# GpSimd instead of VectorE forms two low parts ahead of the first value product

## The chip, the cores and the metric

The kernel runs on one core of one Trainium2 chip. The metric is device time in microseconds; "before" took 577.25 us as the median of three runs (576.12 to 578.04). All data is float32.

## The reference

Three stages follow each other on 4 batches of 768 tokens with 384 features (8 heads of 48). The part that matters here is the start of the second stage, whose input x is the result of the first.

```python
for t in range(S):                                   # stage 1: decayed linear attention
    state = alpha[:, :, t, :, None] * state + np.einsum('bhd,bhe->bhde', k[:, :, t], v[:, :, t])
    y[:, :, t] = np.einsum('bhd,bhde->bhe', q[:, :, t], state)
x = y.transpose(0, 2, 1, 3).reshape(B, S, H * D)

for k in range(K):                                   # stage 2: gate by 5 taps along time, and a value
    gate_pre += conv_w[k][None, None, :] * xp[:, k:k + S, :]
gate = 1.0 / (1.0 + np.exp(-gate_pre))
val = x @ w_val                                      # the product whose operands the change touches
x2 = gate * val @ w_out

u = x2 + np.real(fft(fft(x2, axis=1), axis=2))       # stage 3: Fourier mixing, norm, MLP
un = (u - mean) / np.sqrt(var + 1e-06)
out = u + np.maximum(un @ w_ch1, 0.0) @ w_ch2
```

## The kernel before, in words

Products that need more precision than one pass gives are split. For an operand `a`, ScalarE writes a high part `a_hi` (a copy into the type fp32r), VectorE writes the low part `a_lo = a - a_hi`, and TensorE adds three products: high by high, high by low, low by high. `w_hi`, `w_lo` and `w_raw` hold the weights (`w_lo` lies in the place of `w_raw`), `x_hi` and `x_lo` the input x in two halves of 384 tokens, each 128 partitions by 3 x 384 = 1152 elements.

One list, `SCHEDULE`, sets the order. Every engine walks it and issues its own share of each step; the engines meet only at semaphores, which count. The list is written by hand: `prologue()` for the attention of the first batch, then for each batch `front(b)` (value product, gate, Fourier mixing) and `mlp(b)`, into which the next batch's attention is woven. The attention runs in 6 chunks of 128 tokens. For each chunk VectorE scans the decays forward (`load`, L803) and backward (`inv`, L814), scales k and q (`scale`, L820 and L821, giving `kd` and `qd`), masks the scores that TensorE has made (`mask`, L827) and updates the state (`state`, L835 and L838). TensorE makes the `scores` from `kd` and `qd` (L960), turns the keys (L969), sums the chunk (L980) and forms `y` from the old state (L998) and the masked scores (L1003). ScalarE copies `y` to `xT` (L637).

In `prologue()`, chunk 3 has ScalarE's `whi` of the value weights (L587) and `xhi` of x's first half (L640). VectorE's counterparts come later in its order: `("wlo", 0, 0, 0)` in chunk 4, behind the scales of chunk 5 and the state of chunk 4 (L867), and `("xlo", 0, 0, 0)` in chunk 5, behind that chunk's masks (L870). Between and behind them VectorE adds taps of the gate (`tapv`, L856 and L859). The high and low parts of x's second half follow at chunk 5's end. The first readers are the steps `("val", 0, 0, 0)` and `("val", 0, 1, 0)` of `front(0)` (L1060), which wait for `s_xhi`, `s_xlo` and, for the weights, `s_wlo` through `weight_ready`. `WLO_AT` gives a weight step's number in the count of `s_wlo`.

GpSimd has little to do before: it builds the identity and the mask (L524 to L530), waits until five chunks of x are there, issues the loads of the cosine and sine tables (L536), and then issues all stores (L543). SyncE issues the other loads. TensorE also forms gate taps as products (`tapj`, L1046) and `wd`, the product of the output weights with a Fourier matrix (L1052).

Of the kernel before, what the change touches and what calls it, by code (L numbers as in the profile page):

```python
# [5 lines left out]
F32 = mybir.dt.float32  # L6
F32R = mybir.dt.float32r
ALU = mybir.AluOpType
# [9 lines left out]
HALF = S // 2  # L18
# [4 lines left out]
PAD = TAPS - 1  # L23
# [180 lines left out]
def order_of(*kinds):  # L204

    return {w: j for j, w in enumerate(w for w in SCHEDULE if w[0] in kinds and not (w[0] == "pair" and w[2] > 0))}
# [8 lines left out]
            for w, j in order_of("val", "u", "vlo", "oddrow", "pair", "comb", "t", "h", "out").items()}  # L215
for b_ in range(B):
    DREAD_AT["pqe", b_, 0, 0] = DREAD_AT["pqo", b_, 0, 0]
WHI_AT, WLO_AT = order_of("whi"), order_of("wlo")

def bank_plan():
# [35 lines left out]
def build(nc, q, k, v, alpha, w_val, conv_wt, w_out, w_out_t, w1, w2, dft_d, fold_cos, fold_nsin, odd_col, odd_row, out):  # L257
    ctx = ExitStack()
    with ctx:
        def sb(name, shape, dt=F32):  # L260
            return ctx.enter_context(nc.sbuf_tensor(name, shape, dt))

        def sem(name):
            return ctx.enter_context(nc.semaphore(name))
# [9 lines left out]
        def at(name, shape, dt, offset):  # L274
            return nc.alloc_sbuf_tensor_at(name, shape, dt, offset=offset)
# [3 lines left out]
        w_hi, w_lo, w_raw = {}, {}, {}  # L279
# [12 lines left out]
        x_hi = [at(f"x_hi{h}", [128, K, HALF], F32R, z1 + (2 - 2 * h) * HALFB) for h in range(2)]  # L292
        x_lo = [at(f"x_lo{h}", [128, K, HALF], F32R, z1 + (3 - 2 * h) * HALFB) for h in range(2)]
# [13 lines left out]
        def slot(t):  # L307

            m, mirrored = divmod(t, 2)
            return 2 * m + 2 if mirrored else max(2 * m - 1, 0)  # L310
# [34 lines left out]
        xT = sb("xT", [128, K, PAD + S])  # L345
# [39 lines left out]
        def part(t, i, j):  # L385

            if WN[i] == "w1":
                return t[:, :, j * FF // 3:(j + 1) * FF // 3]
            if WN[i] == "w2":
                return t[:, j, :]  # L390
            return t[:, :, :].rearrange("p k n -> p (k n)")
# [25 lines left out]
        s_diag = sem("diagonals_ready")  # L417
        s_whi = sem("weights_hi")
        s_wlo = sem("weights_lo")

        s_in = [sem("qk_loaded_even"), sem("qk_loaded_odd")]
        s_ain = [sem("alpha_loaded_even"), sem("alpha_loaded_odd")]
# [17 lines left out]

        s_xhi = sem("x_hi_ready")
        s_xlo = sem("x_lo_ready")
        s_tap = sem("taps_added")
        s_tap0 = sem("first_tap_ready")
        s_tapv = sem("first_batch_taps_added")
# [26 lines left out]
        def read(w):  # L472
            return DREAD_AT[w] + 1
# [48 lines left out]
        @block.gpsimd  # L522
        def _(pool):
            pool.memset(ident[:, :], 0.0).then_inc(s_zero, 1)  # L524
            pool.wait_ge(s_zero, 1)
            pool.affine_select(out=ident[:, :], in_=ident[:, :], compare_op=ALU.not_equal, fill=1.0, base=0,
                               pattern=[[-1, 128]], channel_multiplier=1).then_inc(s_consts, 1)
            pool.wait_ge(s_sets, 6)

            pool.affine_select(out=mask[:, :], in_=mask[:, :], compare_op=ALU.is_ge, fill=0.0, base=0,  # L530
                               pattern=[[1, 128]], channel_multiplier=-1).then_inc(s_consts, 1)

            pool.wait_ge(s_xc, NCH - 1)
            for name, table in (("cos", fold_cos), ("nsin", fold_nsin)):
                for dst, part_ in ((w_hi[name], 0), (w_lo[name], 1)):
                    pool.dma_start(dst[:, :, :], table[part_]).then_inc(s_wload[WN.index(name)], 16)  # L536

            for w in SCHEDULE:
                kind, b, a, f = w
                if kind == "out":  # L540
                    t = a * TG + f
                    pool.wait_ge(s_read, read(w))
                    pool.dma_start(out[b, t], u[:, slot(t), :]).then_inc(s_out, 16)  # L543
            pool.wait_ge(s_out, 16 * STORES * B)
# [3 lines left out]
        def _(act):  # L548
# [19 lines left out]
            for w in SCHEDULE:  # L568
                kind, b, a, f = w
# [61 lines left out]
                elif kind == "y":  # L631
                    act.wait_ge(s_y, b * NCH + a + 1)
                    if a == 0 and b > 0:
                        wait_for(act, s_tap, (b - 1) * 2 * (TAPS - 1) * K)
                        act.wait_ge(s_xlo, 2 * b)
                    here = slice(PAD + a * CH, PAD + (a + 1) * CH)
                    act.activation(xT[:, :, here], ys[:, :, :], ACT.Copy).then_inc(s_xc, 1)  # L637
                elif kind == "xhi":
# [48 lines left out]
        def _(dve):  # L687
# [102 lines left out]
            for w in SCHEDULE:  # L790
                kind, b, a, f = w
# [58 lines left out]
                elif kind == "tapv":  # L850
# [6 lines left out]
                    else:  # L857
                        dve.wait_ge(s_tapv, a * TAPS + f)
                        dve.scalar_tensor_tensor(acc, xT[:, m, first + f:end + f], wconv[:, m, f:f + 1], acc,  # L859
                                                 ALU.mult, ALU.add).then_inc(s_tapv, 1)  # L860
                elif kind == "wlo":
                    dve.wait_ge(s_whi, WHI_AT["whi", 0, a, f] + 1)
                    raw, high, low = (part(w_[WN[a]], a, f) for w_ in (w_raw, w_hi, w_lo))
                    if WN[a] == "wout":
                        dve.scalar_tensor_tensor(low, raw, 0.5, high.bitcast(F32), ALU.mult, ALU.subtract).then_inc(s_wlo, 1)
                    else:
                        dve.tensor_tensor(low, raw, high.bitcast(F32), ALU.subtract).then_inc(s_wlo, 1)  # L867
                elif kind == "xlo":
                    dve.wait_ge(s_xhi, 2 * b + a + 1)
                    dve.tensor_tensor(x_lo[a][:, :, :], xT[:, :, PAD + a * HALF:PAD + (a + 1) * HALF],  # L870
                                      x_hi[a][:, :, :].bitcast(F32), ALU.subtract).then_inc(s_xlo, 1)
# [53 lines left out]
        def _(pe):  # L925
# [20 lines left out]
            def weight_ready(name, j=0):  # L946

                pe.wait_ge(s_wlo, WLO_AT["wlo", 0, WN.index(name), j] + 1)
# [77 lines left out]
            for w in SCHEDULE:  # L1026
                kind, b, a, f = w
# [32 lines left out]
                elif kind == "val":  # L1060
                    if a == 0:
                        pe.wait_ge(s_xhi, 2 * b + f + 1)
                        pe.wait_ge(s_xlo, 2 * b + f + 1)
                    if w == ("val", 0, 0, 0):
                        weight_ready("wval")
                    product(ps[:, 0:HALF], [(w_hi["wval"][:, k_, cols], w_lo["wval"][:, k_, cols],
                                             x_hi[f][:, k_, :], x_lo[f][:, k_, :]) for k_ in range(K)]).then_inc(s_unit, 1)
                elif kind == "u":
# [168 lines left out]
```

## Time and profile before

| | before |
|---|---|
| median of 3 runs | 577.25 us (576.12 to 578.04) |
| the profiled execution, its time | 579.33 us |
| its span, first to last instruction | 577.5 us |
| TensorE (PE) busy | 556.3 us |
| VectorE (DVE) busy | 387.9 us |
| ScalarE (ACT) busy | 211.8 us |
| GpSimd (POOL) busy | 16.2 us |
| mean granted TensorE clock | 0.99 |

All times inside the kernel are microseconds from the start of the span. A row of a timeline gives the start, the duration, the engine, the line of the kernel, the operation, output and inputs, the shape, the count of merged instructions, and in brackets the idle time of the engine before it with what ended it. "PEld" is TensorE's weight load, "issue" time without a wait that the profile shows. TensorE's instruction ends are modelled, so its rows overlap; starts are the safer numbers. The granted clock is a share of 2.4 GHz: 1.00 is 2.4 GHz and 0.50 is 1.2 GHz.

### The profile page before, as it was taken

To read this page: it belongs to the slowest core of one execution; us is meant where nothing else is said; L and a number is where in the kernel's file an instruction comes from. 1 tells how busy PE (TensorE), PEld (TensorE's weight loads), DVE (VectorE), ACT (ScalarE), POOL (GpSimd) and SP (SyncE) were. 2 spreads that over 40 slices of the span, in tenths; PEclk is the share of its full clock that TensorE was granted. 3 is DMA by queue.
4 is the path that set the end of the run, shared out by engine and by line. 5 is a ranking of instruction groups with operands and counts; after the bars stand their busy time and mean duration, and the time that the engine had idled before them with its cause. 6 is when DMAs were issued, how large, how long until landed. Compare 5 with 4: busy or idle time off the path is not lost.

```text
span 577.5 us, 13430 instructions
## 1 busy us (share of the span) xinstructions
PE 556.3 (96%) x5623; PEld 530.0 (92%) x5623; DVE 387.9 (67%) x858; ACT 211.8 (37%) x482; POOL 16.2 (3%) x35
## 2 busy tenths in 40 slices
PE   5999999999999999999999999999999999999995
PEld 4887998899999998998999999999999999999995
DVE  7798888978848686877847476886935474552221
ACT  5354364534352135335252134335334134322210
POOL 0001000000000000000000000000000000000000
PEclk9699999999999999999999999999999999999999
DMA  7668301232302000222202001132000000000000
GB/s 254 190 217 294 99 14 44 72 93 63 92 30 57 29 15 28 75 59 86 59 28 59 28 1 42 32 89 87 15 1 28 28 0 2 1 1 28 27 1 27
DMA packets 16234, 34.60 MB, mean 60 GB/s; under 512 B 3312, under 2 KB 6640, under 8 KB 15920
## 3 DMA queue, kind: packets, MB, share of 16 engines
q1 hardware_dynamic: 13632, 27.20, 15.8%
q0 software_dynamic: 2112, 6.29, 3.1%
q8 instruction: 44, 0.72, 0.5%
q10 hardware_dynamic: 432, 0.27, 0.1%
q14 instruction: 14, 0.11, 0.1%
HBM read 29.03 MB, written 4.72 MB: 58 GB/s over the span
## 4 chain that ended last, share of the span: by engine, by line
PE 84%; DVE 7%; ACT 4%; issue 2%; DMA 1%; DVEq 0%; POOL 0%; ACTq 0%
PE bank L933 41%; PE bank L1018 23%; PE evens L960 3%; PE bank L1003 3%; PE bank L998 2%; PE bank L1046 2%; PE sums L969 2%; PE bank L1117 2%; PE sums L980 1%; PE bank L1083 1%; PE bank L1127 1%; PE bank L1052 1%; DVE w_lo L867 1%; DMA oddr_raw<-in_odd_row_dram 1%; DVE unT_lo L690 1%
## 5 line engine op out<-in xcount | busy, mean ns | idle before, releaser
L915 DVE SCALAR_TENSOR_TENSOR h_lo<-bank,h_hi 128x256 fp32r<-128x256 f32 x144 | 60.5, 422 | 106.6 <-ACT h_hi L683 102.1
L933 PE MATMUL bank<-unT_hi,w_hi 128*128 128x256 f32 x432 | 125.1, 290 | 4.5 <-DVE unT_lo L690 2.4
L933 PE MATMUL bank<-unT_lo,w_hi 128*128 128x256 f32 x432 | 122.0, 283 | 0.0
L933 PE MATMUL bank<-unT_hi,w_lo 128*128 128x256 f32 x432 | 121.6, 281 | 0.0
L683 ACT ACTIVATE h_hi<-bank 128x256 fp32r<-128x256 f32 x144 | 54.7, 381 | 164.0 <-PE bank L933 164.0
L1018 PE MATMUL bank<-w_hi,h_hi 128*128 128x384 f32 x288 | 99.9, 347 | 0.0
L1018 PE MATMUL bank<-w_lo,h_hi 128*128 128x384 f32 x288 | 97.6, 339 | 0.0
L1018 PE MATMUL bank<-w_hi,h_lo 128*128 128x384 f32 x288 | 97.3, 338 | 0.0
L933 PEld LDWEIGHTS bank<-unT_hi,w_hi 128*128 128x128 f32 x432 | 81.2, 188 | 9.6 <-DVE unT_lo L690 5.0
L933 PEld LDWEIGHTS bank<-unT_hi,w_lo 128*128 128x128 f32 x432 | 81.6, 189 | 0.0
L933 PEld LDWEIGHTS bank<-unT_lo,w_hi 128*128 128x128 f32 x432 | 81.5, 189 | 0.0
L1018 PEld LDWEIGHTS bank<-w_hi,h_hi 128*128 128x128 f32 x288 | 54.1, 188 | 2.2 <-issue 0.4
L1018 PEld LDWEIGHTS bank<-w_lo,h_hi 128*128 128x128 f32 x288 | 54.1, 188 | 0.0
L1018 PEld LDWEIGHTS bank<-w_hi,h_lo 128*128 128x128 f32 x288 | 54.1, 188 | 0.0
L848 DVE SCALAR_TENSOR_TENSOR gate<-xT,wconv,gate 128x384 f32<-128x384 f32 x72 | 42.3, 611 | 0.4
L960 PEld LDWEIGHTS evens<-qd,kd 48*128 48x128 f32 x192 | 24.0, 193 | 6.8 <-issue 5.1
L814 DVE TENSOR_TENSOR_SCAN kd<-a_in,ends 128x516 f32<-128x516 f32 x24 | 29.6, 1233 | 0.8
L960 PE MATMUL evens<-qd,kd 48*128 48x128 f32 x192 | 28.6, 291 | 1.5 <-DVE qd L821 1.4
L803 DVE TENSOR_TENSOR_SCAN lam<-a_in,starts 128x516 f32<-128x516 f32 x24 | 29.4, 1224 | 0.9 <-DMA a_in<-in_alpha_dram 0.8
L960 PE MATMUL odds<-qd,kd 48*128 48x128 f32 x192 | 28.6, 291 | 0.0
L543 POOL DMA_DIRECT2D out_dram<-u x24 | 12.9, 541 | 513.2 <-DVE u L921 513.2
L1003 PE MATMUL bank<-scores,v_in 128*32 128x128 f32 (+1 forms) x768 | 26.7, 282 | 0.0
(185 smaller groups left out, 1043.4 us busy)
## 6 DMA issues: line engine op xcount, KB each, us to landing
v_in<-in_v_dram SPq DMA_DIRECT2D x24, 224.0 KB, 2.7
w_raw<-in_w_dram SPq DMA_DIRECT2D x2, 2304.0 KB, 10.5
out_dram<-u POOLq DMA_DIRECT2D x24, 192.0 KB, 2.3
a_in<-in_alpha_dram SPq DMA_DIRECT2D x44, 96.9 KB, 2.2
q_in<-in_q_dram SPq DMA_DIRECT2D x44, 96.0 KB, 2.2
k_in<-in_k_dram SPq DMA_DIRECT2D x44, 96.0 KB, 2.3
dftd<-in_dft_d_dram SPq DMA_DIRECT2D x1, 582.0 KB, 4.4
wval_raw<-in_w_val_dram SPq DMA_DIRECT2D x1, 576.0 KB, 5.5
```

The costliest lines, as they stand in the source:

```text
L543: pool.dma_start(out[b, t], u[:, slot(t), :]).then_inc(s_out, 16)
L683: act.activation(h_hi[:, f % HBUF, :], ps[:, 0:GW], ACT.Relu).then_inc(s_hi, 1)
L803: dve.tensor_tensor_scan(lam_[:, :, :].rearrange("d p t -> d (p t)"), a_t[:, 0:NP * CW], starts[:, :, :].rearrange("d p t -> d (p t)"), 0. ...
L814: dve.tensor_tensor_scan(kd_[:, :, :].rearrange("d p t -> d (p t)")[:, ::-1], a_t[:, NP * CW:0:-1], ends[:, NP * CW:0:-1], 0.0, ALU.mult, ...
L848: dve.scalar_tensor_tensor(acc, xT[:, m, t + a * HALF:t + (a + 1) * HALF], wconv[:, m, t:t + 1], acc, ALU.mult, ALU.add).then_inc(s_tap, 1)
L915: dve.scalar_tensor_tensor(h_lo[:, f % HBUF, :], ps[:, 0:GW], 0.0, h_hi[:, f % HBUF, :].bitcast(F32), ALU.max, ALU.subtract).then_inc(s_re ...
L933: last = pe.matmul(ps, l, r, start=(i == 0), stop=(i == len(mms) - 1))
L960: last = pe.matmul(ps[:, p, :], kd_[rows, p, 1:CW], qd_[rows, p, :], start=True, stop=True)
L969: last = pe.transpose(sums[:, p, :], tokens(kd_)[:, p, :], ident[:, :])
L998: pe.matmul(ys[32 * p:32 * p + 32, x, :], st[:, p, first:first + width], qd_[:, p, :], start=(x == 0), stop=False, skip_group_check=True)
L1003: last = pe.matmul(ys[32 * p:32 * p + width, x, :], v_[:, p, first:first + width], scores[:, e, p, :], start=(c == 0 and x == 0), stop=Tru ...
L1018: last = pe.matmul(ps, l[:, f % HBUF, rows], r, start=(f == 0 and x == 0), stop=(f == NF - 1 and x == 2))
```

## The change

The two steps `("wlo", 0, 0, 0)` and `("xlo", 0, 0, 0)` leave VectorE. GpSimd issues the same two subtractions of 128 x 1152 elements right after its mask and ahead of its wait for the table loads: the first when `s_whi` reaches 1, the second when `s_xhi` reaches 1. Each has a semaphore of its own (`s_vallo`, `s_xlo0`), since the counts of `s_wlo` and `s_xlo` are now without them; `WLO_AT` leaves the one step out, and the waits for `s_xlo` count one less. The first val product waits for the two new semaphores in place of the old ones. All other low parts stay with VectorE.

```diff
--- before.py
+++ after.py
@@ -215,7 +215,8 @@
             for w, j in order_of("val", "u", "vlo", "oddrow", "pair", "comb", "t", "h", "out").items()}
 for b_ in range(B):
     DREAD_AT["pqe", b_, 0, 0] = DREAD_AT["pqo", b_, 0, 0]
-WHI_AT, WLO_AT = order_of("whi"), order_of("wlo")
+WHI_AT = order_of("whi")
+WLO_AT = {w: j for j, w in enumerate(w for w in order_of("wlo") if w != ("wlo", 0, 0, 0))}
 
 
 def bank_plan():
@@ -417,6 +418,7 @@
         s_diag = sem("diagonals_ready")
         s_whi = sem("weights_hi")
         s_wlo = sem("weights_lo")
+        s_vallo = sem("val_weights_lo")
 
         s_in = [sem("qk_loaded_even"), sem("qk_loaded_odd")]
         s_ain = [sem("alpha_loaded_even"), sem("alpha_loaded_odd")]
@@ -440,6 +442,7 @@
 
         s_xhi = sem("x_hi_ready")
         s_xlo = sem("x_lo_ready")
+        s_xlo0 = sem("first_x_lo_ready")
         s_tap = sem("taps_added")
         s_tap0 = sem("first_tap_ready")
         s_tapv = sem("first_batch_taps_added")
@@ -529,6 +532,13 @@
 
             pool.affine_select(out=mask[:, :], in_=mask[:, :], compare_op=ALU.is_ge, fill=0.0, base=0,
                                pattern=[[1, 128]], channel_multiplier=-1).then_inc(s_consts, 1)
+
+            pool.wait_ge(s_whi, WHI_AT["whi", 0, 0, 0] + 1)
+            val_raw, val_hi, val_lo = (part(w_["wval"], 0, 0) for w_ in (w_raw, w_hi, w_lo))
+            pool.tensor_tensor(val_lo, val_raw, val_hi.bitcast(F32), ALU.subtract).then_inc(s_vallo, 1)
+            pool.wait_ge(s_xhi, 1)
+            pool.tensor_tensor(x_lo[0][:, :, :], xT[:, :, PAD:PAD + HALF], x_hi[0][:, :, :].bitcast(F32),
+                               ALU.subtract).then_inc(s_xlo0, 1)
 
             pool.wait_ge(s_xc, NCH - 1)
             for name, table in (("cos", fold_cos), ("nsin", fold_nsin)):
@@ -632,7 +642,7 @@
                     act.wait_ge(s_y, b * NCH + a + 1)
                     if a == 0 and b > 0:
                         wait_for(act, s_tap, (b - 1) * 2 * (TAPS - 1) * K)
-                        act.wait_ge(s_xlo, 2 * b)
+                        act.wait_ge(s_xlo, 2 * b - 1)
                     here = slice(PAD + a * CH, PAD + (a + 1) * CH)
                     act.activation(xT[:, :, here], ys[:, :, :], ACT.Copy).then_inc(s_xc, 1)
                 elif kind == "xhi":
@@ -858,14 +868,14 @@
                         dve.wait_ge(s_tapv, a * TAPS + f)
                         dve.scalar_tensor_tensor(acc, xT[:, m, first + f:end + f], wconv[:, m, f:f + 1], acc,
                                                  ALU.mult, ALU.add).then_inc(s_tapv, 1)
-                elif kind == "wlo":
+                elif kind == "wlo" and w in WLO_AT:
                     dve.wait_ge(s_whi, WHI_AT["whi", 0, a, f] + 1)
                     raw, high, low = (part(w_[WN[a]], a, f) for w_ in (w_raw, w_hi, w_lo))
                     if WN[a] == "wout":
                         dve.scalar_tensor_tensor(low, raw, 0.5, high.bitcast(F32), ALU.mult, ALU.subtract).then_inc(s_wlo, 1)
                     else:
                         dve.tensor_tensor(low, raw, high.bitcast(F32), ALU.subtract).then_inc(s_wlo, 1)
-                elif kind == "xlo":
+                elif kind == "xlo" and (b, a) != (0, 0):
                     dve.wait_ge(s_xhi, 2 * b + a + 1)
                     dve.tensor_tensor(x_lo[a][:, :, :], xT[:, :, PAD + a * HALF:PAD + (a + 1) * HALF],
                                       x_hi[a][:, :, :].bitcast(F32), ALU.subtract).then_inc(s_xlo, 1)
@@ -1060,9 +1070,11 @@
                 elif kind == "val":
                     if a == 0:
                         pe.wait_ge(s_xhi, 2 * b + f + 1)
-                        pe.wait_ge(s_xlo, 2 * b + f + 1)
-                    if w == ("val", 0, 0, 0):
-                        weight_ready("wval")
+                        if (b, f) == (0, 0):
+                            pe.wait_ge(s_xlo0, 1)
+                            pe.wait_ge(s_vallo, 1)
+                        else:
+                            pe.wait_ge(s_xlo, 2 * b + f)
                     product(ps[:, 0:HALF], [(w_hi["wval"][:, k_, cols], w_lo["wval"][:, k_, cols],
                                              x_hi[f][:, k_, :], x_lo[f][:, k_, :]) for k_ in range(K)]).then_inc(s_unit, 1)
                 elif kind == "u":
```

## Rows read from the trace of the kernel before

**Rows 1.** The page: busy time of each engine, then the chain's shares by engine.
```profile
PE 556.3 (96%) x5623; PEld 530.0 (92%) x5623; DVE 387.9 (67%) x858; ACT 211.8 (37%) x482; POOL 16.2 (3%) x35
...
PE 84%; DVE 7%; ACT 4%; issue 2%; DMA 1%; DVEq 0%; POOL 0%; ACTq 0%
```

**Rows 2.** Waits of 10 to 60 us: us in total, times, longest.
```profile
PE sums L980 <- ACT kdT L630: 4.9, 2, 4.1
...
DVE x_lo L870 <- ACT x_hi L640: 1.4, 1, 1.4
```

**Rows 3.** Timeline of VectorE, 34.5 to 52 us: start, duration, line, operands.
```profile
35.44 1.23 DVE L803 TENSOR_TENSOR_SCAN lam<-a_in,starts 128x516 f32<-128x516 f32 x1
...
37.02 1.27 DVE L859 SCALAR_TENSOR_TENSOR gate<-xT,wconv,gate 128x384 f32<-128x384 f32 x2
38.20 0.69 DVE L827 TENSOR_TENSOR scores<-evens,mask 128x512 f32<-128x512 f32 x1
38.80 0.68 DVE L827 TENSOR_TENSOR scores<-odds,mask 128x512 f32<-128x512 f32 x1
...
39.61 1.23 DVE L814 TENSOR_TENSOR_SCAN kd<-a_in,ends 128x516 f32<-128x516 f32 x1
...
41.54 0.68 DVE L821 TENSOR_TENSOR qd<-q_in,lam 128x512 f32<-128x512 f32 x1
...
42.91 1.35 DVE L867 TENSOR_TENSOR wval_lo<-wval_raw,wval_hi 128x1152 fp32r<-128x1152 f32 x1
44.18 1.26 DVE L859 SCALAR_TENSOR_TENSOR gate<-xT,wconv,gate 128x384 f32<-128x384 f32 x2
...
46.56 1.35 DVE L870 TENSOR_TENSOR x_lo<-xT,x_hi 128x1152 fp32r<-128x1152 f32 x1
...
51.69 1.36 DVE L870 TENSOR_TENSOR x_lo<-xT,x_hi 128x1152 fp32r<-128x1152 f32 x1 [1.44 <-ACT x_hi L640]
```

**Rows 4.** Timeline of TensorE, 38 to 75 us.
```profile
42.65 1.06 PE L1003 MATMUL bank<-scores,v_in 128*32 128x128 f32 x32
43.64 0.37 PE L960 MATMUL evens<-qd,kd 48*128 48x128 f32 x1
...
53.19 0.35 PE L933 MATMUL bank<-x_hi,wval_hi 128*128 128x384 f32 x1
...
64.73 0.41 PE L1083 MATMUL bank<-wd_hi,dif_hi 128*128 128x388 f32 x1 [0.23 <-issue]
```

**Rows 5.** Timeline of ScalarE, 24 to 42 us.
```profile
34.05 1.17 ACT L587 ACTIVATE wval_hi<-wval_raw 128x1152 fp32r<-128x1152 f32 x1
35.12 1.15 ACT L640 ACTIVATE x_hi<-xT 128x1152 fp32r<-128x1152 f32 x1
```

**Rows 6.** Timeline of GpSimd, 0 to 110 us.
```profile
3.07 0.29 POOL L530 TENSOR_SCALAR_AFFINE_SELECT mask<-mask 128x128 f32<-128x128 f32 x1 [1.54 <-DVE xT L787]
44.57 0.69 POOL L536 DMA_DIRECT2D cos_hi<-in_fold_cos_dram  x1 [41.21 <-ACT xT L637]
```

**Rows 7.** Groups of VectorE by shape, 35 to 53 us: count, busy us, mean ns.
```profile
L859 DVE SCALAR_TENSOR_TENSOR gate<-xT,wconv,gate 128x384 f32<-128x384 f32 x4 | 2.5, 616 | 0.1
L859 DVE SCALAR_TENSOR_TENSOR gate<-xT,wconv,gate 128x256 f32<-128x256 f32 x4 | 1.9, 484 | 0.1
...
L856 DVE TENSOR_SCALAR gate<-xT,wconv 128x384 f32<-128x384 f32 x2 | 0.8, 404 | 0.0
...
L856 DVE TENSOR_SCALAR gate<-xT,wconv 128x256 f32<-128x256 f32 x1 | 0.3, 347 | 0.0
```

**Rows 8.** Stretches: busy of PE, PEld, DVE, ACT, POOL, clock, DMA share, GB/s.
```profile
12.00:14.00 2.00, 0.07 (x5) 0.10 (x9) 1.30 (x3) 1.88 (x8) 0.00 (x0) 0.74 0.93 344
...
22.00:24.00 2.00, 2.00 (x48) 1.79 (x41) 1.97 (x4) 0.16 (x1) 0.00 (x0) 0.70 0.58 142
```

**Rows 9.** The chain in order of time, 13 to 30 us.
```profile
21.20 1.28 PE bank L998 x24
...
28.16 0.66 PE bank L998 x24
```

## The prediction

> **What bounds the kernel now.** I read the page's busy shares and chain first. TensorE (PE) is busy for 556.3 of 577.5 us and carries 84% of the chain; VectorE (DVE) carries 7% [rows 1]. So work taken from VectorE is worth something only where TensorE waits for VectorE. The change acts between about 35 and 55 us, so I then read the waits of 10 to 60 us: TensorE's large wait there, 4.9 us in two pieces, is for a ScalarE copy before 20.5 us, and VectorE itself waits 1.4 us for the high part of x's second half [rows 2]. The order in time shows the rest. The two VectorE instructions that go stand at 42.91 and 46.56 us [rows 3]; their readers are the first val products, which start at 53.19 us [rows 4]. From 42.65 us to 56 us TensorE runs without a gap over 0.1 us in its timeline. Within this stretch VectorE is far ahead of its own wait at 51.69 us, where it stands idle for 1.44 us [rows 3].
>
> **What is removed, and what that gives back.** Two subtractions over 128x1152, each 1.35 us long, leave VectorE. From start to start the first takes 44.18 - 42.91 = 1.27 us; the second has the same shape, so 2.54 us in all. (Start to start is shorter than the duration because VectorE begins the next instruction before the last one has drained.) Where do 2.54 us go? Everything between 42.91 and 51.69 moves up, and then VectorE waits for x_hi's second half, which ScalarE makes from TensorE's product. The idle 1.44 us becomes 1.44 + 2.54 = 3.98 us. Nothing after 51.69 us starts earlier. The next place where TensorE waits for VectorE is 0.23 us at 64.73 us [rows 4], behind the queue that starts at 51.69, so it stays. The removal is worth 0. Its upper bound is those 0.23 us, the only pause of TensorE from 42 to 65 us for which VectorE could be the cause.
>
> **What is added on GpSimd (POOL), and when it runs.** wval_hi is ready at 34.05 + 1.17 = 35.22 us and x_hi's first half at 35.12 + 1.15 = 36.27 us [rows 5]. GpSimd has been idle since its mask at 3.07 us, which started 0.07 us after its releaser. So the first subtraction wants to start at 35.3 us and the second directly after it. Its length: no two-tensor GpSimd instruction is in the trace. The nearest row of the same engine is the mask's select, 0.29 us for 128 elements per partition from one tensor [rows 6]; nine times that, for 1152, is an estimate of 2.6 us. The lower end is VectorE's 1.35 us, the upper end twice 2.6 = 5.2 us, if each tensor costs a pass. I take 2.6, because the row is of that engine. Both results are then there by 35.3 + 2 x 2.6 = 40.5 us undisturbed, 12.7 us before TensorE reads them at 53.19; even with 5.2 each it is 45.7 us. That they come too late is ruled out short of 8.9 us each. Behind them on GpSimd's queue stand the four table loads (cosine and sine), issued from 44.57 us at up to 0.69 us each [rows 6]. GpSimd is free before 44.57 us at 2.6 us each and 1.1 us late at 5.2; the tables are first read behind the products that start at 64.73 us. Cost 0 either way. SyncE's queue is not touched, and the stores on GpSimd come at 125 us and later. TensorE's waits are changed one for one, and ScalarE's wait before the second batch only counts one less. Cost 0.
>
> **What GpSimd does to VectorE: the term that decides.** From 35.3 us on GpSimd reads and writes SBUF in 1152-element streams, beside a VectorE that is busy without a pause and mostly reads two SBUF tensors. The trace has no such pair, so I bound it. Lower end: no effect, 0. The only neighbours in the trace are the table loads from 44.57 us, beside which the two-tensor instructions of VectorE keep their durations [rows 3, 6]; but these read no tensor. Upper end: every VectorE instruction with two SBUF tensors waits for the whole of the GpSimd instruction. 
>
> The Trainium skill, "SBUF — State Buffer", section "SBUF: two separate sides", speaks against this change: the second pair of ports belongs to VectorE and GpSimd in turn, as an exclusive lock for a whole instruction, also against a VectorE instruction with two SBUF inputs. No row of before shows it. By the length in "GPSIMD Engine Reference", section "Performance versus the Vector engine" (4497 ns for a two-input add of 2048 elements), each subtraction would be an estimate of 2.5 us, and the sum below would be less by under 0.2 us.
>
> Worked out for the upper end. VectorE's `lam` scan would start at 35.44 [rows 3]. The first GpSimd instruction holds it until 35.3 + 2.6 = 37.9, a delay of 2.46 us. The second follows at the next gap in VectorE's queue, for 2.6 more: 5.06 us. If the second falls on the two mask instructions at 38.20 and 38.80, which read PSUM and one SBUF tensor and may run beside it, up to 39.61 - 38.20 = 1.4 us of it are hidden: 3.65 us. What is late next? TensorE's `y` product at 42.65 needs the mask that ended at 38.80 + 0.68 = 39.48, a slack of 3.2 us. The `scores` of chunk 5 at 43.64 [rows 4] need `qd`, which ended at 41.54 + 0.68 = 42.22; 0.13 us must lie between them, so the slack is 1.3 us. Delay minus slack: 5.06 - 1.3 = 3.8 us, or 3.65 - 1.3 = 2.4 us. TensorE has no idle time behind it to give this back, so it stays to the end of the kernel. VectorE then catches up, because the 2.54 us that it lost are gone from its queue, so the masks of chunk 5 are not a second loss.
>
> **The sum.** The profiled execution took 579.33 us around a span of 577.5, and the median of the runs is 577.25. The change adds the same 3.8 us to each: span 581.3, that execution 583.1, median 577.25 + 3.8 = 581.0 us. I take the upper of the two values, since two gaps in VectorE's queue (before the scaled adds at 37.02) come ahead of the masks.
>
> **Rivals.**
> Case A, the forecast: GpSimd holds up VectorE, TensorE loses 2.4 to 3.8 us: 579.6 to 581.3 us. Chance 0.45.
> Case B, slower by the clock as well. TensorE's pauses at 42.65 and 43.64 sum to 3.8 us with 1 us of work between them. The trace has one pause of this size: idle for 4.1 us up to 13.93 us [rows 2], after which the granted clock is at 0.50 (1.2 of 2.4 GHz) until some point of 22 to 24 us [rows 8] (the first and the last of six such stretches). The same 24 products take 1.28 us at that level and 0.66 us at the full one [rows 9]. By the means of 0.74 and 0.70 the clock was low for 1.0 us of 12 to 14 and 1.2 us of 22 to 24, with the 8 us between them some 10 us; half of that is 5 us lost at most. 577.25 + 3.8 + 3 to 5 = 584 to 586 us. Against it: the pauses are divided. Chance 0.10. It decides from the point at which the two pauses act as one.
> Case C, GpSimd needs 5.2 us for each: delay 2 x 5.2 - 0.1 = 10.3, less 1.3: 9.0, or 586.3 us. Chance 0.03.
> Case D, no contention: GpSimd has a path of its own, or waits itself until VectorE is idle. VectorE's queue then keeps its times up to 42.91 us, and the change is worth nothing: 577.3 us. For it: the durations beside the table loads. Chance 0.28.
> Case E, contention that finds the slack: GpSimd gets its turns on the masks and behind `qd` only. Delay at `qd` 2.6 - 1.4 = 1.2 us, under the slack of 1.3: 577.3 us. Or its instructions are as short as VectorE's 1.35: 2 x 1.35 - 0.1 - 1.3 = 1.3 us, 578.6. Chance 0.10.
> Case F, faster: only if VectorE's queue up to 64.73 us were tied to the removed 2.54 us by something that the rows don't show. The gap itself gives 0.23 us; the whole 2.54 us would give 574.7 us. Chance 0.04.
>
> **How the numbers follow.** About 0.3%, 1.7 us, is what a measurement of this kernel can tell from no change. Slower by more: A, B, C, 0.58. Within: D and E, 0.38. Faster: 0.04. The time is that of A, 581.0. The range reaches down over D and E to 576.7 and up to 583.5, which covers A with 2 us for lengths between 2.6 and 5.2; B, C and F, 0.17, are left out. A alone has 579.5 to 582.5, D and E 576.7 to 578.6.
>
> **What would show it.** Right: two GpSimd subtractions from 35.3 us; in the same microseconds VectorE instructions that are longer than 1.23 or 0.63 us, or gaps before them without a releaser, 3.5 to 5 us in sum by `qd`; `qd` of chunk 5 ending at 46 to 47.3 us instead of 42.22; TensorE waiting for the masks of chunk 4 and for `qd`; the first val product at about 57.0 instead of 53.19; everything after it moved by the same amount; VectorE's idle time before x_lo's second half about 4 us where the clock and the queue allow. Wrong: VectorE's durations between 35 and 41 us unchanged beside GpSimd's instructions (D), GpSimd's instructions themselves stretched or late (D, E), or granted clock under 1.00 between 44 and 56 us (B). The forecast fails if the two engines read SBUF side by side, or if GpSimd's share of the turns falls behind 42.2 us.

## The result, and the profile after

The changed kernel takes 585.0 us (median of 4 runs, 584.78 to 586.13), the kernel before beside it 577.64 us. The ratio is 1.0128, with a 95% interval of 1.0107 to 1.0150: 7.4 us slower. The profiled execution has a span of 583.1 us.

The page of the changed kernel: busy time of each engine, and the shares of the chain. They answer to [rows 1]; VectorE's share of the chain went from 7% to 11%.

```profile
PE 558.2 (96%) x5623; PEld 530.5 (91%) x5623; DVE 390.2 (67%) x856; ACT 212.3 (36%) x482; POOL 21.5 (4%) x37
...
PE 80%; DVE 11%; ACT 4%; issue 3%; DMA 1%; DVEq 0%; POOL 0%; ACTq 0%
```

ScalarE and GpSimd in order of time, answering to [rows 5] and [rows 6]. GpSimd's subtractions take 2.63 and 2.75 us (estimated: 2.6).

```profile
32.60 1.17 ACT L597 ACTIVATE wval_hi<-wval_raw 128x1152 fp32r<-128x1152 f32 x1
```
```profile
33.85 2.63 POOL L538 TENSOR_TENSOR wval_lo<-wval_raw,wval_hi 128x1152 fp32r<-128x1152 f32 x1 [30.49 <-ACT wval_hi L597]
36.45 2.75 POOL L540 TENSOR_TENSOR x_lo<-xT,x_hi 128x1152 fp32r<-128x1152 f32 x1
```

In this execution the stretch stands earlier than in that of [rows 5], by 34.05 - 32.60 = 1.45 us. It goes with a shorter low clock near the start: 0.50 up to about 18 us here, up to about 23 us there. So positions are compared after taking off 1.45. VectorE's rows ahead of GpSimd's first instruction then stand 0.15 us late already (`qd` of chunk 4 at 32.88 us instead of 34.18 - 1.45 = 32.73). VectorE in order of time, answering to [rows 3]:

```profile
33.86 2.83 DVE L848 TENSOR_TENSOR state<-state_new,fin 128x192 f32<-128x192 f32 x1
36.62 3.66 DVE L813 TENSOR_TENSOR_SCAN lam<-a_in,starts 128x516 f32<-128x516 f32 x1
...
41.81 0.68 DVE L837 TENSOR_TENSOR scores<-evens,mask 128x512 f32<-128x512 f32 x1
...
45.15 0.68 DVE L831 TENSOR_TENSOR qd<-q_in,lam 128x512 f32<-128x512 f32 x1
...
56.95 1.36 DVE L880 TENSOR_TENSOR x_lo<-xT,x_hi 128x1152 fp32r<-128x1152 f32 x1 [5.23 <-ACT x_hi L650]
```

The state update, normally 0.36 us, lasts 2.83 us and ends 0.2 us behind GpSimd's first instruction. The scan, normally 1.23 us, lasts 3.66 and ends about one scan's length behind GpSimd's second. `qd` starts at 45.15 instead of 41.54 - 1.45 = 40.09: a delay of 5.06 us. GpSimd's own share is (2.83 - 0.36) + (3.66 - 1.23) = 4.9 us, the rest is the 0.15 us from above. TensorE in order of time, answering to [rows 4]:

```profile
43.15 1.19 PE L1013 MATMUL bank<-scores,v_in 128*32 128x128 f32 x32 [1.76 <-DVE scores L837]
45.98 0.55 PE L970 MATMUL evens<-qd,kd 48*128 48x128 f32 x1 [1.64 <-DVE qd L831]
...
58.46 0.35 PE L943 MATMUL bank<-x_hi,wval_hi 128*128 128x384 f32 x1
```

Two new pauses, 1.76 and 1.64 us. The scores of chunk 5 start at 45.98 instead of 43.64 - 1.45 = 42.19: 3.79 us late. But the first val product, at 58.46 instead of 53.19 - 1.45 = 51.74, is 6.72 us late. The stretches tell where the other 2.93 us went (columns as in [rows 8], the clock third from the right):

```profile
45.00:46.00 1.00, 0.02 (x2) 0.05 (x2) 1.00 (x3) 0.00 (x0) 0.83 (x2) 0.62 0.00 0
46.00:48.00 2.00, 2.00 (x17) 1.78 (x17) 1.61 (x4) 0.72 (x2) 1.47 (x3) 0.50 0.70 183
48.00:50.00 2.00, 2.00 (x5) 1.16 (x4) 1.87 (x4) 0.00 (x0) 0.00 (x0) 0.50 1.17 382
50.00:52.00 2.00, 2.00 (x4) 1.01 (x3) 1.62 (x4) 0.00 (x0) 0.00 (x0) 0.50 0.66 226
52.00:53.00 1.00, 1.00 (x10) 0.97 (x9) 0.00 (x0) 0.49 (x1) 0.00 (x0) 0.97 0.03 9
```

Behind the pauses the granted clock is at 0.50 (1.2 GHz) from about 45.2 to 52 us. Before, it was 1.00 there. From 45.98 us on TensorE has work for all of this stretch, and that work takes longer: 12.48 us from the scores to the val product instead of 9.55.

### The profile page after: what moved, and what is told of

It is laid out like the page before. It is cut to its first block, busy times and chain, and to the rows that moved or that the text cites. A ratio compares the mean times of both kernels' runs of the same rounds, so it can differ in the third digit from the quotient of the medians.

```text
span 583.1 us, 13430 instructions
## 1 busy us (share of the span) xinstructions
PE 558.2 (96%) x5623; PEld 530.5 (91%) x5623; DVE 390.2 (67%) x856; ACT 212.3 (36%) x482; POOL 21.5 (4%) x37
## 4 chain that ended last, share of the span: by engine, by line
PE 80%; DVE 11%; ACT 4%; issue 3%; DMA 1%; DVEq 0%; POOL 0%; ACTq 0%
PE bank L943 41%; PE bank L1028 23%; PE evens L970 3%; PE bank L1013 3%; PE bank L1008 2%; PE bank L1129 2%; PE bank L1095 1%; PE bank L1139 1%; PE sums L979 1%; DVE lam L813 1%; PE bank L1062 1%; DVE kd L824 1%; PE sums L990 1%; DVE w_lo L877 1%; DVE scores L837 1%
## 5 line engine op out<-in xcount | busy, mean ns | idle before, releaser
L813 DVE TENSOR_TENSOR_SCAN lam<-a_in,starts 128x516 f32<-128x516 f32 x24 | 31.8, 1326 | 1.0 <-DMA a_in<-in_alpha_dram 1.0
```

The source lines that it names most:

```text
L813: dve.tensor_tensor_scan(lam_[:, :, :].rearrange("d p t -> d (p t)"), a_t[:, 0:NP * CW], starts[:, :, :].rearrange("d p t -> d (p t)"), 0. ...
```

## The experiments

Each profile gives one number that the drifting start of an execution doesn't disturb: the distance from the start of `wval_hi` on ScalarE to the first val product on TensorE. Before, it is 53.19 - 34.05 = 19.14 us. The table gives how much longer it is in each kernel, beside what the runs say ("in us" is the ratio turned into microseconds of the kernel before). There is one profile of each kernel, two of the changed one.

| kernel | distance longer by | ratio to before (95%) | in us | clock of 44 to 52 us |
|---|---|---|---|---|
| changed | 6.72 | 1.0128 (1.0107 to 1.0150) | +7.4 | falls to 0.50 |
| e11_changed_again | 6.71 | 1.0127 (1.0110 to 1.0144) | +7.3 | falls to 0.50 |
| e1_filled | 3.67 | 1.0078 (1.0049 to 1.0106) | +4.5 | 1.00 |
| e5_fill_first | 3.80 | 1.0086 (1.0063 to 1.0110) | +5.0 | 1.00 |
| e12_fill_second | 3.80 | 1.0080 (1.0063 to 1.0097) | +4.6 | 1.00 |
| e9_in_thirds | 3.55 | 1.0102 (1.0087 to 1.0117) | +5.9 | falls to 0.50 |
| e2_weights_only | 1.30 | 1.0029 (1.0018 to 1.0041) | +1.7 | 1.00 |
| e7_one_tensor | 0.81 | 1.0021 (1.0005 to 1.0037) | +1.2 | 1.00 |
| e8_on_masks | 0.14 | 1.0010 (0.9996 to 1.0024) | +0.6 | 1.00 |
| e3_later_turns | 0.00 | 1.0015 (1.0002 to 1.0027) | +0.9 | 1.00 |
| e6_writes_only | 0.00 | 1.0009 (0.9998 to 1.0020) | +0.5 | 1.00 |
| e4_left_out | 0.01 | 1.0008 (0.9996 to 1.0021) | +0.5 | 1.00 |
| e10_busy_start | 0.00 | 1.0013 (0.9995 to 1.0031) | +0.7 | 1.00 |

The two columns of microseconds follow each other but for e9. Every other kernel reads 0.4 to 1.2 us more in time than in distance, those without a loss too. The profiles show a part of it outside this distance: from the first val product to the end of the span it is 524.3 us before and 524.2 to 525.0 in the others, and the time is 1.8 us longer than the span before and 1.7 to 2.2 in the others. In e9 the excess is 2.3 us, of which 0.4 lie behind the val product and 0.2 outside the span. The rest was not taken apart; ahead of `wval_hi`, where nothing was changed, executions differ by the length of their low clock (6.8 to 13.7 us in these profiles, 3.4 in e10).

**Is the loss behind the pauses the clock's? (e1_filled)** The changed kernel with products that nobody reads, in both pauses (the comments are added here):

```diff
+                if n == 5:                       # ahead of the wait for qd
+                    for _ in range(7):
+                        pe.matmul(bank[0][:, 0:128], ident[:, :], ident[:, :], start=True, stop=True)
...
+                if n == 4:                       # ahead of the wait for the masks
+                    for _ in range(7):
+                        pe.matmul(bank[0][:, 0:128], ident[:, :], ident[:, :], start=True, stop=True)
```

> The changed kernel, with 7 products of 128x128 that nobody reads put on TensorE ahead of its wait for the masks of chunk 4, and 7 more ahead of its wait for `qd` of chunk 5. At full clock one takes some 0.22 us (the gate taps: 2.23 us for 10), so 1.5 us fit into each of the two pauses (1.76 and 1.64 us) without moving what follows. Theory (the pauses cost 3.8 us themselves, and 2.9 us more is the clock that falls behind them): the granted clock stays at 1.00 from 40 to 56 us, the pauses' end times stay, and the time is 585.0 - 2.9 = about 582 us. Rival (the loss behind the pauses is not the clock's but belongs to the delayed order of work): no gain, 585 us or a little more.

Measured 582.54 us against 577.92, +4.5. TensorE in order of time (the trace counts two instructions for each of these products, so 7 of them are x14), then its stretch of 44 to 46 us:

```profile
39.76 1.83 PE L1015 MATMUL bank<-ident 128*128 128x128 f32 x14
41.52 1.08 PE L1019 MATMUL bank<-scores,v_in 128*32 128x128 f32 x32
42.53 1.83 PE L967 MATMUL bank<-ident 128*128 128x128 f32 x14
44.29 0.37 PE L973 MATMUL evens<-qd,kd 48*128 48x128 f32 x1
...
53.85 0.34 PE L943 MATMUL bank<-x_hi,wval_hi 128*128 128x384 f32 x1
```
```profile
44.00:46.00 2.00, 2.00 (x22) 1.62 (x21) 1.93 (x6) 0.72 (x2) 1.76 (x4) 1.00 0.55 111
```

The pauses are full of idle work, and the clock stays up. The delay of the val product is 3.67 us, that of the pauses alone. By the ratios, work that nobody reads makes the changed kernel 2.9 us faster (7.4 - 4.5). The theory stands. VectorE's rows in this execution show who waits for whom a second time:

```profile
32.57 3.66 DVE L813 TENSOR_TENSOR_SCAN lam<-a_in,starts 128x516 f32<-128x516 f32 x1
36.16 2.75 DVE L866 TENSOR_SCALAR gate<-xT,wconv 128x384 f32<-128x384 f32 x1
```
```profile
32.29 2.85 POOL L538 TENSOR_TENSOR wval_lo<-wval_raw,wval_hi 128x1152 fp32r<-128x1152 f32 x1 [28.93 <-ACT wval_hi L597]
35.09 3.58 POOL L540 TENSOR_TENSOR x_lo<-xT,x_hi 128x1152 fp32r<-128x1152 f32 x1
```

The scan is held until GpSimd's first instruction has ended; GpSimd's second then waits for the scan (3.58 us instead of 2.75); and then the first tap product, which reads one SBUF tensor only, is held: 2.75 us instead of the 0.40 of [rows 7]. The engines take turns, one instruction each.

**One subtraction instead of two (e2_weights_only).** The x subtraction goes back to VectorE, and so do the counts that hang on it (not shown):

```diff
-            pool.wait_ge(s_xhi, 1)
-            pool.tensor_tensor(x_lo[0][:, :, :], xT[:, :, PAD:PAD + HALF], ...).then_inc(s_xlo0, 1)
```

> GpSimd makes only the low part of the value weights; VectorE makes that of x's first half, as before. Theory (VectorE's two-tensor instruction is held for the whole of GpSimd's one, 2.6 us, of which 1.3 us are slack up to `qd`): the pause ahead of the scores of chunk 5 is some 1.1 to 1.3 us, too short for the clock to fall: 577.6 + 1.2 = 578.8 us. Rival (loss in proportion, each subtraction bears half of the 7.4 us): 581.3 us.

Measured 579.64 us, +1.7 (1.0 to 2.4). VectorE, then TensorE:

```profile
34.99 3.66 DVE L810 TENSOR_TENSOR_SCAN lam<-a_in,starts 128x516 f32<-128x516 f32 x1
```
```profile
44.36 0.34 PE L967 MATMUL evens<-qd,kd 48*128 48x128 f32 x1 [1.23 <-DVE qd L828]
```

The scan is held by 2.4 us, of which 1.2 us reach TensorE. The rival's 3.7 us are excluded. Two subtractions cost over four times as much as one: the slack of 1.3 us is spent on half of the first, the second is paid in full, and then the clock falls.

**Is the stretch or the reading at fault? (e3_later_turns)** Both subtractions on GpSimd, started later:

```diff
+            pool.wait_ge(s_qd, NCH)
             pool.wait_ge(s_whi, WHI_AT["whi", 0, 0, 0] + 1)
...
+            pool.wait_ge(s_mask, 2 * NCH)
             pool.wait_ge(s_xhi, 1)
```

> Both subtractions stay on GpSimd, but the first starts only when `qd` of chunk 5 is there and the second only when the masks of chunk 5 are there. VectorE has a wait of its own at the end of that stretch. Theory (what costs is the turn that falls ahead of `qd`): the state of chunk 4 is held for 2.6 us within a slack of some 3 us, the second falls on taps that nobody waits for; clock 1.00, time 577 to 578 us as the kernel before. Rival (GpSimd's reading beside VectorE costs wherever it stands): 580 us or more.

Measured 578.66 us, ratio 1.0015. VectorE is held nearly as long:

```profile
41.23 2.63 DVE L850 TENSOR_TENSOR state<-state_new,fin 128x192 f32<-128x192 f32 x1
...
46.53 4.32 DVE L871 SCALAR_TENSOR_TENSOR gate<-xT,wconv,gate 128x256 f32<-128x256 f32 x4
```

The state update takes 2.63 instead of 0.36 us and the four taps 4.32 instead of 2.04. That is 4.55 us in sum, against 4.9 in the changed kernel. TensorE doesn't notice up to the val product: the distance is 19.14 us, as before. Behind it, its next pause (0.23 us in [rows 4]) is 0.44 us here. The rival (it costs 2 us or more wherever it stands) falls.

**What is the removal worth? (e4_left_out)**

```diff
-            pool.tensor_tensor(val_lo, val_raw, val_hi.bitcast(F32), ALU.subtract).then_inc(s_vallo, 1)
...
+            pool.memset(x_lo[0][:, :, :].bitcast(F32), 0.0).then_inc(s_xlo0, 1)      # at the start
...
-                    product(ps[:, 0:HALF], [(w_hi["wval"][:, k_, cols], w_lo["wval"][:, k_, cols],
+                    product(ps[:, 0:HALF], [(w_hi["wval"][:, k_, cols], w_hi["wval"][:, k_, cols],
```

> Neither engine makes the two low parts: the low part of x's first half is filled with zeros at the start of the kernel, and the value product reads the high part of the weights in place of the low one. This is the price of the two subtractions on VectorE by itself. Theory: VectorE's freed 2.54 us only lengthen its wait for the second half of x_hi; 577.6 us, as before. Rival (VectorE's queue bounds the stretch by a path that the rows don't show): up to 575.1 us.

Measured 578.33 us, ratio 1.0008 (0.9996 to 1.0021): the removal is worth nothing that can be measured, even if nobody does the work (the output then lacks these parts). VectorE's row shows where its time goes:

```profile
50.62 1.36 DVE L875 TENSOR_TENSOR x_lo<-xT,x_hi 128x1152 fp32r<-128x1152 f32 x1 [3.16 <-ACT x_hi L645]
```

The wait of [rows 3] grows by 3.16 - 1.44 = 1.7 us (the masks of chunk 5 now wait 0.67 us for their scores, which takes most of the rest of the 2.54).

**What does GpSimd's instruction have to do to hold VectorE? (e6_writes_only, e7_one_tensor)** Both are the kernel before, with two extra GpSimd instructions of 1152 elements at the moment of `wval_hi`. The extract is shortened: the second instruction waits for the first, and VectorE's `x_lo` for both.

```diff
+            pool.wait_ge(s_whi, 1)
+            pool.memset(x_lo[0][:, :, :].bitcast(F32), 0.0).then_inc(s_x0free, 1)             # e6, twice
+            pool.tensor_copy(x_lo[0][:, :, :], xT[:, :, PAD:PAD + HALF]).then_inc(s_x0free, 1)  # e7, twice
```

> The kernel before, in which GpSimd from the moment of wval_hi on writes zeros twice into the place of x_lo's first half (1152 elements, no tensor read); VectorE makes both low parts itself, as before. Theory (GpSimd's reading takes VectorE's second read path; an instruction that only writes takes none): VectorE's two-tensor instructions keep 1.23, 0.63 and 0.69 us, and the time is 577.9 us. Rival (any GpSimd instruction on SBUF holds VectorE): the `lam` scan or its neighbour is lengthened by the length of a GpSimd write.

Measured 578.04 us, ratio 1.0009. GpSimd, then VectorE:

```profile
34.16 1.06 POOL L535 MEMSET x_lo<- 128x1152 f32 x1 [30.81 <-ACT wval_hi L592]
35.28 1.06 POOL L537 MEMSET x_lo<- 128x1152 f32 x1
```
```profile
34.33 1.23 DVE L808 TENSOR_TENSOR_SCAN lam<-a_in,starts 128x516 f32<-128x516 f32 x1
35.47 1.07 DVE L861 TENSOR_SCALAR gate<-xT,wconv 128x384 f32<-128x384 f32 x1
```

The scan, with two tensors, runs beside both writes in its usual 1.23 us. The tap product with one tensor (0.45 ns an element when alone, by the prediction's reading of [rows 7]) lasts 1.07 instead of 0.40 us and ends 0.2 us behind the second write. Half of the theory holds: the scan, a two-tensor instruction, isn't held by a GpSimd instruction that only writes. The rival is right about the neighbour, which is held until the write ends, and wrong in its reason, since the scan goes free.

> As e6, but GpSimd copies x's first half to the place of x_lo twice: one tensor of 1152 elements read, one written. Theory: VectorE's two-tensor instructions are held for GpSimd's whole length, and this length is shorter than 2.6 us if the two tensors of a subtraction share one read path; with about 1.3 us each, a delay of at most 2.6 us and a pause of 1.3 us on TensorE: 578 to 579.2 us. Rival (only an instruction with two tensors collides): VectorE's durations stay, 577.9 us.

Measured 578.76 us, ratio 1.0021. GpSimd's first copy, then VectorE, then TensorE:

```profile
33.30 1.15 POOL L535 CAST x_lo<-xT 128x1152 fp32r<-128x1152 f32 x1 [29.95 <-ACT wval_hi L592]
```
```profile
33.34 1.33 DVE L843 TENSOR_TENSOR state<-state_new,fin 128x192 f32<-128x192 f32 x1
34.59 2.17 DVE L808 TENSOR_TENSOR_SCAN lam<-a_in,starts 128x516 f32<-128x516 f32 x1
```
```profile
42.46 0.34 PE L967 MATMUL evens<-qd,kd 48*128 48x128 f32 x1 [0.73 <-DVE qd L826]
```

One tensor read is enough: the state update is held by 0.97 us and the scan by 0.94. The rival falls. A copy takes 1.15 us, a subtraction 2.63: the second tensor more than doubles the length on GpSimd.

**Which VectorE instructions are free? (e8_on_masks)** The first subtraction waits for the third tap step, the second for the masks of chunk 5:

```diff
+            pool.wait_ge(s_tapv, 3)
             pool.wait_ge(s_whi, WHI_AT["whi", 0, 0, 0] + 1)
...
+            pool.wait_ge(s_mask, 2 * NCH)
             pool.wait_ge(s_xhi, 1)
```

> Both subtractions on GpSimd; the first starts when three tap steps are done, which is when VectorE comes to the masks of chunk 4 (they read PSUM and one SBUF tensor), the second when the masks of chunk 5 are there. Theory (VectorE is held only where it uses both of its read paths on SBUF): the two masks and the reciprocal keep 0.69, 0.68 and 0.17 us beside GpSimd, the backward scan behind them is held for the remaining 1.2 us, which is under the slack of 1.3 us, and TensorE shows no pause: 577.9 to 578.7 us. Rival (every VectorE instruction is held, PSUM or not): the first mask is lengthened by 2.6 us, the pause ahead of `qd` is 1.2 us as in e2: 579.6 us.

Measured 577.91 us, ratio 1.0010. GpSimd's first instruction, from 35.96 to 38.61 us, and beside it VectorE:

```profile
35.96 2.65 POOL L539 TENSOR_TENSOR wval_lo<-wval_raw,wval_hi 128x1152 fp32r<-128x1152 f32 x1 [32.60 <-DVE gate L871]
```
```profile
35.79 0.68 DVE L839 TENSOR_TENSOR scores<-evens,mask 128x512 f32<-128x512 f32 x1
36.39 0.68 DVE L839 TENSOR_TENSOR scores<-odds,mask 128x512 f32<-128x512 f32 x1
36.99 0.17 DVE L824 RECIPROCAL ends<-lam 128x4 f32<-128x4 f32 x1
37.20 2.50 DVE L826 TENSOR_TENSOR_SCAN kd<-a_in,ends 128x516 f32<-128x516 f32 x1
```

The masks, which read one tensor from PSUM, keep their 0.68 us, and the second of them starts and ends while GpSimd's instruction runs. So does the reciprocal, which reads one SBUF tensor of 4 elements: 0.17 us, as before. Not every instruction on SBUF alone is held, then; which property separates it from the tap product was not tried. The scan behind them is held by 2.50 - 1.23 = 1.27 us; the slack takes nearly all of it, and the distance grows by 0.14 us.

**Smaller pieces (e9_in_thirds).** Each subtraction as three of 384 elements:

```diff
-            pool.tensor_tensor(val_lo, val_raw, val_hi.bitcast(F32), ALU.subtract).then_inc(s_vallo, 1)
+            for k_ in range(K):
+                pool.tensor_tensor(w_lo["wval"][:, k_, :], w_raw["wval"][:, k_, :],
+                                   w_hi["wval"][:, k_, :].bitcast(F32), ALU.subtract).then_inc(s_vallo, 1)
```

> The changed kernel, with each GpSimd subtraction issued as three of 384 elements. Theory (the two engines take turns, a whole instruction each; e1, e5 and the changed kernel show one VectorE instruction between GpSimd's two): six turns of some 0.9 us, with a VectorE instruction in each gap; those that fall beside the masks of chunk 4 cost nothing, so the delay at `qd` is 3.5 to 5 us, the pauses of TensorE 2.2 to 3.7 us, and the time 580 to 582 us with the clock up, 585 if it falls. Rival (GpSimd keeps the path while it has work queued): as the changed kernel, VectorE's state update or scan held for 2.6 us at once.

Measured 582.9 us, ratio 1.0102. VectorE, then TensorE, then its clock:

```profile
34.83 2.03 DVE L815 TENSOR_TENSOR_SCAN lam<-a_in,starts 128x516 f32<-128x516 f32 x1
36.78 1.08 DVE L868 TENSOR_SCALAR gate<-xT,wconv 128x384 f32<-128x384 f32 x1
37.90 2.51 DVE L871 SCALAR_TENSOR_TENSOR gate<-xT,wconv,gate 128x384 f32<-128x384 f32 x2
```
```profile
44.88 0.34 PE L972 MATMUL evens<-qd,kd 48*128 48x128 f32 x1 [1.78 <-DVE qd L833]
```
```profile
46.00:47.00 1.00, 1.00 (x4) 0.60 (x3) 1.00 (x2) 0.16 (x1) 0.27 (x1) 0.69 1.07 344
47.00:48.00 1.00, 1.00 (x3) 0.63 (x2) 1.00 (x3) 0.00 (x0) 0.00 (x0) 0.50 1.15 378
...
49.00:50.00 1.00, 1.00 (x5) 0.69 (x4) 0.93 (x3) 0.11 (x1) 0.00 (x0) 0.61 1.03 359
```

Turns again: 0.8 us more on the scan, 0.7 on the tap product, 1.2 on the two taps. The fifth and sixth pieces run beside the masks, and the sixth ends at 42.26 us within the backward scan, which it holds by another 0.4 us (41.73 us, 1.62 long). The sum is 3.1 us at `qd`. Alone, a piece takes 1.09 us (the first) and 1.02 us (the last), more than a third of 2.63, so cutting up costs GpSimd time. The masks are in time, so only one pause is left, and the scores are 1.85 us late. The clock falls all the same: at about 46.4 us, 1.5 us behind the end of the pause and in the midst of work, and for 3.4 us. That costs the other 1.7 us of the distance. The time, 0.9 us above the expected 580 to 582 with the clock up, lies between the two cases.

**How long a pause does it take? (e5_fill_first, e12_fill_second)** As e1, with one of its two blocks of products.

> As e1, but only the pause ahead of the masks of chunk 4 is filled with 7 unread products; the pause of some 1.6 us ahead of `qd` stays empty. Theory (the two pauses together, 3.4 us idle of 4.6, made the clock fall; one of 1.7 us does not, as the 1.2 us of e2 did not): granted clock 1.00 from 40 to 56 us and 577.9 + 4.5 = 582.4 us, as e1. Rival (any pause of 1.6 us or more lets it fall): 585 us.

Measured 582.49 us, +5.0, clock 1.00. The pause that was to stay empty moved: 1.25 us inside the `y` product and 0.24 us ahead of the scores. So this run doesn't test a single pause of 1.6 us.

```profile
44.11 0.93 PE L1016 MATMUL bank<-scores,v_in 128*32 128x128 f32 x25 [1.25 <-issue]
45.27 0.34 PE L970 MATMUL evens<-qd,kd 48*128 48x128 f32 x1 [0.24 <-DVE qd L831]
```

> As e5 the other way round: the pause ahead of the masks of chunk 4 (1.5 to 1.8 us) stays empty, that ahead of `qd` is filled with 7 unread products. Theory by now (e9's one pause of 1.8 us was followed by the low clock, the pauses of 1.2 us in e2 and of 1.25 and 0.24 us in e5 were not: a single pause near 1.8 us can be enough): the clock at 0.50 for some us between 43 and 52, 584 to 585 us. Rival (the clock falls only behind both pauses, e9's fall had another reason): clock 1.00 and 582 us as e1 and e5.

Measured 582.41 us, +4.6. The pause ahead of `y` is as long as in the changed kernel, and the clock stays at 1.00 from 36 to 60 us:

```profile
42.37 1.08 PE L1016 MATMUL bank<-scores,v_in 128*32 128x128 f32 x32 [1.77 <-DVE scores L837]
```

The theory missed here. With either pause filled, the loss behind the pauses is gone; with both open it is there, in both profiles of the changed kernel. But e9 has one pause of 1.78 us and the fall, e12 one of 1.77 us and none. The moment differs too: in the changed kernel's two profiles the clock falls within the second pause (at 45.2 and 45.7 us) and is low for 6.8 us, in e9 it falls behind the pause and is low for 3.4 us. The length of a pause alone doesn't decide. What else does stays open.

**Once more, and the start of the kernel (e11_changed_again, e10_busy_start).** The first is the changed kernel unaltered; the second the kernel before with 16 unread products ahead of the first chunk sum.

> The changed kernel as it is, once more beside these. Theory: GpSimd's instructions of 2.6 and 2.75 us, VectorE's state update and scan held, pauses of 1.8 and 1.6 us, the clock at 0.50 behind them, 585 us. Rival (the fall of the clock is a matter of chance in each execution): 582 us in some of the runs and a profile with the clock at 1.00.

Measured 584.58 us, ratio 1.0127. Here the turns fall as in e1 (the scan 3.66 us, the first tap product 2.74), and the pauses are 1.49 and 1.75 us. The sum is the same: distance 25.85 us. The clock falls again.

> The kernel before (no GpSimd subtraction), with 16 unread products of 128x128 ahead of TensorE's first chunk sum, where it stands idle for some 4 us (9.8 to 13.9 us), after which the clock is at half for 7 to 13 us in every profile so far. Theory (the clock falls behind idle time and a stretch at half clock costs what its work takes more): granted clock 1.00 from 8 to 24 us, and VectorE becomes the bound of a part of the stretch, so 2 to 4 us less: 574 to 576 us. Rival (the low clock at 10 to 24 us is hidden behind VectorE, or does not come from the idle time): 577.6 us.

Measured 577.52 us, ratio 1.0013: no gain. The clock was down to 0.56 and 0.58 in 8 to 10 and 10 to 12 us before the filling could help, so it ran at half clock itself, and 1.00 after 12 us. But the filling also got in the way: the `kdT` that the first chunk sum waits for ends at 12.57 us, and the sum starts only at 14.83 us, behind the unread products. Before, it started 0.15 us behind `kdT` (13.93 us). So the run shows that this filling brings nothing, and not that the low clock costs nothing: up to 14.83 - 12.57 - 0.15 = 2.1 us of gain could be hidden by it. No version here beats the kernel before.

## Why the prediction was right and where it was wrong

The direction was right, and so was the way from GpSimd's instructions to TensorE's two pauses. What the pauses do to the clock was left out of the sum, which gave 3.8 us where 7.4 came. By its steps:

- Removal worth 0: right. e4 measures +0.5 us with an interval that spans zero. VectorE's idle time ahead of x_lo's second half is 5.23 us in the changed kernel, more than the 3.98 forecast, because x_hi itself came 6.72 us late and VectorE's queue only 5.06 (3.98 + 6.72 - 5.06, less 0.41 us of waiting ahead of the masks of chunk 5).
- GpSimd's length 2.6 us each: 2.63 and 2.75. Nothing behind it on its queue suffered; the tables were issued at 45.17 us, when released.
- VectorE is held for whole instructions: right, with 5.06 us of delay at `qd` as computed, though by other instructions. That it is the same to the hundredth is luck, since 0.15 us of it were there before GpSimd began. The prediction had GpSimd win twice within VectorE's scan and taps; the rows show strict turns, one VectorE instruction between GpSimd's two, and it is the same for the sum which ones they are. The reading of [rows 7], that two-tensor instructions use both of VectorE's read paths and GpSimd takes one of them, fits e7, where one read tensor holds them, and e6, where none does not. It doesn't cover e6's tap product, held by a GpSimd instruction that reads nothing.
- Slack of 1.3 us and loss of 3.8 us at the scores: 3.79 us; with the clock kept up (e1) 3.67 us.
- The escape over the masks (case E): real. e8 shows it with 1.27 us of delay against the 1.2 computed. In the changed kernel no GpSimd instruction reached them.
- The clock: this is the step that failed. The sum took the pauses at their length, with the granted clock at 1.00 behind them; it was at 0.50 for 6.8 us, which cost 2.9 us more. The fall stood as case B with 584 to 586 us, and 585.0 is what came. It had a chance of 0.10, on the single argument that the two pauses are divided, and the range ended at 583.5, below it. The one comparable row, the 4.1 us pause of [rows 2], could not say how much less is enough, so no row spoke for a chance as low as 0.10. The term of B itself, 3 to 5 us (no row gives its lower end), measured 2.9 (6.72 - 3.79 = 2.93 in the profile; 7.4 - 4.5 = 2.9 between the changed kernel and e1). That the time falls in the middle of case B is luck in part. The sum 3.8 + 2.9 = 6.7 us leaves 0.7 us of the 7.4, of which 0.3 us is in the profile between the val product and the end (5.6 us of span + 1.45 - 6.72).

## What to carry to other kernels

GpSimd isn't a free engine beside a busy VectorE: ask of each elementwise step moved there which VectorE instructions stand in the same microseconds, and whether their tensors all lie in SBUF. Here it was free beside the masks, which read PSUM, and within VectorE's slack. And price a new pause of TensorE twice, once for its length and once for the clock that may fall behind it. A reserve of slack, here 1.3 us, is what a move has to be measured against, before any busy share.

## What the runs showed of the hardware

- GpSimd and VectorE take turns by whole instructions, also where both have several queued (the changed kernel, e1, e9). A GpSimd subtraction holds a VectorE instruction with two SBUF tensors (0.36 to 2.83 us, 1.23 to 3.66 us) and the tap product with a single one (0.40 to 2.75 us), and neither the masks, which read PSUM (0.68 us), nor the reciprocal of 4 elements (0.17 us, e8). The Trainium skill, "SBUF — State Buffer", section "SBUF: two separate sides", calls the port pair that the two share an exclusive lock, held for the whole instruction. The traces agree for the instructions with two SBUF tensors. It adds that two SBUF inputs collide only with a GpSimd instruction that reads SBUF: e6 agrees, the scan keeps 1.23 us beside a write.
- Not expected: a GpSimd instruction that only writes holds VectorE's one-tensor instruction (0.40 to 1.07 us in e6).
- For 1152 elements GpSimd takes 1.06 us to fill, 1.15 us to copy and 2.63 us to subtract two tensors (a longer row holds a wait for VectorE: 2.75 to 3.58 us); VectorE subtracts in 1.35 us. For 384 elements GpSimd takes 1.02 to 1.09 us where it doesn't wait (e9).
- Not expected: pauses of TensorE of 1.76 and 1.64 us, divided by a product of some 1.2 us, went with 6.8 us at half clock, from within the second of them on; one pause of 1.77 us (e12) was followed by none, and one of 1.78 us (e9) by 3.4 us, from 1.5 us behind its end.
